# Retention, feed-forward and expert attention in one kernel: pair 0 loaded over two queues, pairs 1 and 2 scaled by GpSimd, and the last pair's mask ahead of low parts

## The chip, the cores and the metric

The kernel runs on one core of a Trainium2 chip. The metric is device time in microseconds (us), the median of several executions. A core has five engines that run their own instruction streams and meet at semaphores: TensorE (PE in the profile), VectorE (DVE), ScalarE (ACT), GpSimd (POOL) and SyncE (SP), which only issues transfers here. PEld are TensorE's weight loads. A name with q (SPq, ACTq) is an engine's own queue of issued transfers.

## The reference, cut to what matters

```python
# 1. retention: q, k, v are (2, 8, 768, 64)
gamma = 1.0 - 2.0 ** (-5.0 - np.arange(H))
for t in range(S):
    state = gamma * state + k[:, :, t] (outer) v[:, :, t]
    y[:, :, t] = 1 / sqrt(D) * q[:, :, t] @ state
# 2. feed-forward on x = y as (2, 768, 512)
xn = (x - mean) / sqrt(var + 1e-6) * g_ln
x = x + relu(xn @ w_ch1) @ w_ch2              # 512 -> 2048 -> 512
# 3. four attention experts, the best two of four by x @ w_gate
for e in range(4):
    a = softmax(causal(scale * (x @ wq[e]) @ (x @ wk[e]).T))
    out += weight_of(e) * (a @ (x @ wv[e]) @ wo[e])
```

The decay of the retention is moved into q and k: row t of q is multiplied by gamma^t / sqrt(D) and row t of k by gamma^-t (t counted from the middle), so that the rest is a causal product without decay.

## The kernel before

**Pairs.** The 16 (batch, head) combinations are worked as 8 pairs of two heads (`NIT` = 8, `HP` = 4 of each batch), a pair as 6 chunks of 128 rows in two halves `g` of three chunks. For a pair `it`:

- `load_heads(it)` on SyncE: k, q and v, 384 KB each, into one of three buffers (`RB`). From pair 3 on, k and q wait until the scaling of pair it - 3 is done, and v until its outputs are.
- `scale_rows` (L295): one half of k or q times its column of the table `decay`, a multiplication with two inputs in SBUF. VectorE does pairs 0 and 1 and q of pair 2; GpSimd does the rest in `scale_pair`, in the order k, q of half 0 and k, q of half 1. They wait for `s_tab_rest`, the rest of the table.
- `turn` (TensorE, L614): three transposes for each of four units, k and q of half 0, k and q of half 1, each into a PSUM bank; `turned` (ScalarE, L960) evacuates one unit into `k_t` or `q_t`.
- `scores_of` (L624): 6 products for a half; `apply_causal` (VectorE, L1176) masks them into `prob`.
- `key_values` (L671): k times v of chunks 0 to 4; `states` (VectorE, L1185 and L1188) adds them up, one copy and four additions, each waiting for the one before.
- `chunk_outputs` (L637) and `state_outputs` (L644): both add into the pair's output banks; `y_out` (ScalarE, L966) takes them to `x`, already transposed.

Products in fp32 are two instructions each in the profile, except the transposes. TensorE's order is written out by hand: in steady state scores(it), chunk_outputs(it - 1), key_values(it), state_outputs(it - 1), turn(it + 1).

**Front.** Pair 0 comes in pieces by half and head: `FIRST` is k0, q0, k1, q1, v0, v1, each two pieces of 96 KB. SyncE issues the first table (12 KB), the head-0 pieces of k0 and q0, both pieces of the others, then the rest of the table, which holds seven pairs although the values of both batches are equal, then pair 1. ScalarE issues the head-1 pieces of k0 and q0. TensorE meanwhile does 18 transposes (L677) that nobody reads. VectorE's order is: scale pair 0, `apply_causal(0, 0)`, `states(0)`, `apply_causal(0, 1)`, scale pair 1.

**Into the feed-forward block.** It works in float32r parts, hi and lo of each operand, and takes three of the four products: `PASSES` is (hi, hi), (hi, lo), (lo, hi), the first of each the weight and the second the activation. The inner loop of `hidden` (L727) needs the normalised x: `first_sum` (L1240, L1244) adds the four pairs of a batch into `head_sum`, `first_mean` (TensorE, L654) makes the mean, `first_centre` (L1250) subtracts it, `first_hi` (ScalarE, L978) writes the hi part and `first_lo` (VectorE, L1256) the lo part. `first_centre(b, kk)`, `first_hi` and `first_lo` exist for two batches `b` and four blocks `kk` of 128. Those of batch 0 are done during pairs 6 and 7, those of batch 1 after the last pair. `hidden(0, 0)` waits block by block for the lo part of batch 1.

**Last pairs.** TensorE's order there is scores(7), key_values(7), chunk_outputs of half 0 of pairs 6 and 7, their state_outputs, chunk_outputs of half 1 of both, `first_mean(1)`, state_outputs of half 1 of both, `hidden(0, 0)`. After it come the feed-forward block, in three stages of 16 `hidden` and 16 `project` (L736), and the attention, both in TensorE's hand-written order, up to the end.

Of the kernel before, what the change touches and what calls it, by code (L numbers as in the profile page):

```python
# [32 lines left out]
P = 128  # L33
# [3 lines left out]
FAR = 3e38  # L37


def decay_tables(heads, seq, head_dim, batch):  # L40


    gamma = 1.0 - 2.0 ** (-5.0 - np.arange(heads, dtype=np.float64))
    t = np.arange(seq, dtype=np.float64).reshape(seq // P, P) - seq // 2
    power = gamma[None, None, :] ** t[:, :, None]
    both = np.stack([power / np.sqrt(head_dim), 1.0 / power])
    both = both.reshape(2, seq // P, P, heads // 2, 2).transpose(2, 0, 3, 1, 4)
    both = both.reshape(P, 2, heads // 2, -1)
    return np.concatenate([both] * batch, axis=2).astype(np.float32)


class Chain:
# [18 lines left out]
def retention_moe_program(nc, q, k, v, g_ln, w_ch1, w_ch2, w_gate, wq, wk, wv, wo, out):  # L71
    B, H, S, D = q.shape
    DM, FF = w_ch1.shape
    E = w_gate.shape[1]
    HP = H // 2
    NIT = B * HP
# [8 lines left out]
    G = 3  # L85
# [4 lines left out]
    assert B == 2 and D == 64 and DM == H * D == 512 and NC == 6 and E * D == 2 * P and N == 512  # L90

    heads = {n: a.rearrange("b (i j) (c p) d -> (b i) p j c d", j=2, p=P) for n, a in (("q", q), ("k", k), ("v", v))}
    tables = nc.inline_tensor(decay_tables(H, S, D, B), name="decay")
    w1_rows = w_ch1.rearrange("(k p) f -> p k f", p=P)
    w2_rows = w_ch2.rearrange("(f p) n -> p f n", p=P)
    gate_rows = w_gate.rearrange("(k p) e -> p k e", p=P)
# [5 lines left out]
    with ExitStack() as ctx:  # L102
        def sb(scope, name, shape, dt=F32):
            return scope.enter_context(nc.sbuf_tensor(name, shape, dt))

        def sem(name):
            return ctx.enter_context(nc.semaphore(name))
# [6 lines left out]
        mean_of = sb(ctx, "mean_of", [P, P], F32R)  # L114
        causal = sb(ctx, "causal", [P, P])
        masked = sb(ctx, "masked", [P, NC, P], BF16)
        decay = sb(ctx, "decay_sb", [P, 2, NIT, 2 * NC])
        rvar = sb(ctx, "rvar", [P, NT])
        g_col = sb(ctx, "g_col", [P, KT])

# [80 lines left out]
        s_const = sem("s_const")  # L201
        s_tab, s_tab_rest = sem("s_tab"), sem("s_tab_rest")
        s_wraw, s_gcol = sem("s_wraw"), sem("s_gcol")
        s_first = {n: [sem(f"s_first_{n}{g}") for g in range(2)] for n in "qkv"}
        s_load = {n: [sem(f"s_load_{n}{m}") for m in range(RB)] for n in "qkv"}
        s_scaled = {n: sem(f"s_scaled_{n}") for n in "qk"}

# [33 lines left out]
        s_done = [sem(f"s_done{n}") for n in range(3)]  # L241


        PASSES = (("hi", "hi"), ("hi", "lo"), ("lo", "hi"))

        def f32(ap):
# [32 lines left out]
        def part_of(g):  # L279
            return slice(G * g, G * g + G)  # L280

        FIRST = (("k", 0), ("q", 0), ("k", 1), ("q", 1), ("v", 0), ("v", 1))

        def wait_loaded(engine, n, which, g):

            if n == 0:
                engine.wait_ge(s_first[which][g], 32)
            else:
                engine.wait_ge(s_load[which][n % RB], 16 * (n // RB + (n % RB > 0)))

        def scale_rows(engine, n, which, g):

            wait_loaded(engine, n, which, g)
            factors = decay[:, "qk".index(which), n, 2 * G * g:2 * G * (g + 1)].rearrange("p (c j) -> p c j", j=2)
            engine.tensor_tensor(scaled[which][:, n % RB, part_of(g)].rearrange("p c (j d) -> p c j d", j=2),  # L295
                                 raw[which][:, n % RB, :, part_of(g)].rearrange("p j c d -> p c j d"),
                                 factors.unsqueeze(3).broadcast_to((P, G, 2, D)),
                                 ALU.mult).then_inc(s_scaled[which], 1)
# [101 lines left out]
        def _(sp):  # L400
# [38 lines left out]
                    sp.dma_start(f32(k_twice["lo"][j * D:(j + 1) * D, e % 2, b, cols]),  # L439
                                 f32(pj["lo"][D:2 * D, n % 2, :])).then_inc(s_spread[n % 2], 16)  # L440

            sp.dma_start(decay[:, :, 0:1, :], tables[:, :, 0:1, :]).then_inc(s_tab, 16)
            for n, g in FIRST:
                for j in range(1 if (n, g) in FIRST[0:2] else 2):
                    sp.dma_start(raw[n][:, 0, j, part_of(g)], heads[n][0][:, j, part_of(g)]).then_inc(s_first[n][g], 16)
            sp.dma_start(decay[:, :, 1:NIT, :], tables[:, :, 1:NIT, :]).then_inc(s_tab_rest, 16)
            for it in range(1, NIT):
                load_heads(it)
                if it == RB:
# [26 lines left out]
        def _(pool):  # L476
# [34 lines left out]
            def scale_pair(n):  # L511

                for g in range(2):
                    for which in "kq"[0:1 if n == 2 else 2]:
                        if g == 0 and (n, which) in ((2, "k"), (3, "q")):
                            pool.wait_ge(s_scaled[which], 2 * n)
                        if n == 2 and g == 0:
                            pool.wait_ge(s_tab_rest, 16)
                        if n >= RB and g == 0:
                            pool.wait_ge(s_t, 4 * (n - RB) + 4)  # L520
                            if which == "k":
                                pool.wait_ge(s_kv, n - RB + 1)
                        scale_rows(pool, n, which, g)

            for n in range(2, NIT):
                scale_pair(n)
            split_w1(0)
            split_w1(1)
# [76 lines left out]
        def _(pe):  # L605
# [33 lines left out]

            def state_outputs(it, g):  # L640

                pe.wait_ge(s_st, (NC - 1) * (it + 1))
                for c in range(max(1, G * g), G * g + G):
                    mm = pe.matmul(y_bank(it, g)[:, (c - G * g) * P:(c - G * g + 1) * P], state[:, it % 2, c - 1, :],  # L644
                                   q_t[:, it % 2, c, :], start=False, stop=True, skip_group_check=True)
                mm.then_inc(s_y, 1)
# [28 lines left out]
            pe.wait_ge(s_const, 2)  # L675
            for _ in range(18):
                pe.transpose(ps[:, 5, 0:P], ident[:, :], ident[:, :])  # L677
            for unit in range(4):
                turn(0, unit)
                if unit == 1:  # L680
                    scores_of(0, 0)
            key_values(0)
            scores_of(0, 1)
            for g in range(2):
                chunk_outputs(0, g)
                state_outputs(0, g)
            for unit in range(4):
                turn(1, unit)
            for it in range(1, NIT - 1):

                for g in range(2):
                    scores_of(it, g)
                if it > 1:
                    for g in range(2):
                        chunk_outputs(it - 1, g)
                key_values(it)
                if it > 1:
                    for g in range(2):
                        state_outputs(it - 1, g)
                for unit in range(4):  # L700
                    turn(it + 1, unit)
                if it == HP + 1:
                    first_mean(0)
# [14 lines left out]
            def hidden(i, f):  # L718
                pe.wait_ge(s_w1, f + 1)
                if f >= 2:  # L720

                    pe.wait_ge(s_hlo, NF * i + f - 1)
                for kk in range(KT):
                    if f == 0:
                        pe.wait_ge(s_xlo, KT * (i + 1) + kk + 1)
                    for p_, (a_, b_) in enumerate(PASSES):
                        mm = pe.matmul(ps[:, f % 2, :], w1[a_][:, f, kk, :], xn_t[b_][:, kk, :],  # L727
                                       start=(kk == 0 and p_ == 0), stop=(kk == KT - 1 and p_ == 2))
                mm.then_inc(s_h, 1)
# [221 lines left out]
        def _(act):  # L951
# [31 lines left out]
            act.wait_ge(s_const, 2)  # L983

            act.activation(rvar[:, :], ident[:, 0:NT], ACT.Sqrt).then_inc(s_preload, 1)
            for unit in range(4):
                turned(0, unit)
            for it in range(1, NIT):
                if it == HP + 3:
                    for kk in range(KT):  # L990
                        first_hi(0, kk)
                if it != 2:
                    for g in range(2):
                        y_out(max(0, it - 2), g)
                for unit in range(4):
                    turned(it, unit)
            for it in (NIT - 2, NIT - 1):
                y_out(it, 0)
            for kk in range(KT):
# [169 lines left out]
        def _(dve):  # L1169
# [26 lines left out]
            dve.wait_ge(s_preload, 1)  # L1196
            dve.wait_ge(s_const, 4)
            apply_causal(0, 0)
            states(0)
            apply_causal(0, 1)  # L1200
            dve.wait_ge(s_tab_rest, 16)
            for g in range(2):
                for n in "kq":
                    scale_rows(dve, 1, n, g)

            def normalise(n):

# [142 lines left out]
            for it in range(1, NIT):  # L1350
                if it == HP + 2:
                    for kk in range(KT):
                        first_centre(0, kk)
                if it == HP + 3:
                    for kk in (2, 3):
                        first_lo(0, kk)
                b, kk = divmod(it - 2, HP)
                if it >= 2 and kk > 0:
                    first_sum(b, kk)
                apply_causal(it, 0)  # L1360
                if it < NIT - 1:
                    apply_causal(it, 1)
                if it == 1:
                    for g in range(2):
                        scale_rows(dve, 2, "q", g)
                states(it)
                if it == HP + 2:
                    for kk in (0, 1):
                        first_lo(0, kk)
            apply_causal(NIT - 1, 1)  # L1370
            first_sum(1, HP - 2)
            first_sum(1, HP - 1)
            first_centre(1, 0)
# [191 lines left out]
```

## Time and profile before

| | |
|---|---|
| median of 3 runs | 468.07 us (467.91 to 468.2) |
| the profiled execution | 467.95 us |
| its span, first to last instruction | 466.2 us |
| TensorE busy in the span | 453.8 us, 97% |
| VectorE, ScalarE, GpSimd busy | 272.1, 149.6, 151.9 us |
| granted TensorE clock, mean | 1.00 |

The profile is of one execution. Times in its views count from the start of the span. "Busy" counts an instruction from start to end, and TensorE's overlap, so a busy TensorE is not one without waits; the chain of waits and the timeline tell more. In the timeline [idle before <-releaser] is how long the engine had stood idle and what ended that; rows that follow one another without a pause are merged, with their number behind the x.

### The profile page before, as it was taken

How to read it: one execution, taken by the hardware profiler on the slowest of the kernel's cores; microseconds unless marked ns; L12 is line 12 of the kernel's file. 1: busy time of each engine (PE TensorE's matmuls, PEld its weight loads, DVE VectorE, ACT ScalarE, POOL GpSimd, SP SyncE). 2: the span in 40 equal slices, each digit the busy share in tenths (PEclk: the TensorE clock that was granted, in tenths of full speed). 3: DMA queues.
4: the chain of work that ended last, by engine and by line, in shares of the span. 5: the costliest groups of instructions: out<-in, count | busy, mean ns of one | idle time of the engine just before them, and what ended most of it. 6: DMA issues, size and time to landing. Idle time of an engine off the chain costs nothing.

```text
span 466.2 us, 7435 instructions
## 1 busy us (share of the span) xinstructions
PE 453.8 (97%) x2762; PEld 393.0 (84%) x2762; DVE 272.1 (58%) x601; ACT 149.6 (32%) x343; POOL 151.9 (33%) x188
## 2 busy tenths in 40 slices
PE   7999999999999999999999999999999999999896
PEld 6899888888888888888888888888999899998775
DVE  4765941385416388732265784144538889888833
ACT  2344431111212111111121111141435777777823
POOL 1264449999600000000002000001402567666710
PEclk9999999999999999999999999999999999999999
DMA  7997415444000000000040000000155444442024
GB/s 170 248 218 180 125 46 136 135 135 136 22 1 1 0 0 0 0 0 0 0 112 3 0 1 0 0 2 0 24 136 123 113 123 105 99 105 63 1 112 159
DMA packets 65792, 33.04 MB, mean 71 GB/s; under 512 B 47584, under 2 KB 61920, under 8 KB 65760
## 3 DMA queue, kind: packets, MB, share of 16 engines
q1 hardware_dynamic: 64960, 32.43, 26.9%
q8 instruction: 19, 0.31, 0.3%
q10 hardware_dynamic: 800, 0.20, 0.2%
q14 instruction: 13, 0.11, 0.1%
HBM read 20.03 MB, written 3.15 MB: 50 GB/s over the span
## 4 chain that ended last, share of the span: by engine, by line
PE 86%; DVE 7%; ACT 2%; issue 2%; POOL 1%; DMA 0%; POOLq 0%; ACTq 0%; DVEq 0%
PE ps L727 28%; PE ps L736 28%; PE ps L811 5%; PE ps L862 4%; PE ps L783 3%; PE ps L830 3%; PE ps L845 2%; PE ps L889 2%; PE ps L637 2%; PE ps L624 2%; PE ps L614 2%; DVE a L1445 2%; PE ps L644 2%; DVE a_low_lo L1453 1%; PE ps L677 1%
## 5 line engine op out<-in xcount | busy, mean ns | idle before, releaser
L1296 DVE SCALAR_TENSOR_TENSOR h_t_lo<-ps,h_t_hi 128x512 fp32r<-128x512 f32 x48 | 33.2, 692 | 124.4 <-ACT h_t_hi L1012 124.4
L1012 ACT ACTIVATE h_t_hi<-ps 128x512 fp32r<-128x512 f32 x48 | 28.7, 598 | 216.2 <-PE ps L727 216.2
L727 PE MATMUL ps<-xn_t_hi,w_hi 128*128 128x512 f32 x192 | 74.9, 390 | 0.3 <-DVE xn_t_lo L1256 0.3
L727 PE MATMUL ps<-xn_t_lo,w_hi 128*128 128x512 f32 x192 | 74.8, 390 | 0.0
L727 PE MATMUL ps<-xn_t_hi,w_lo 128*128 128x512 f32 x192 | 74.8, 390 | 0.0
L736 PE MATMUL ps<-w_hi,h_t_lo 128*128 128x512 f32 x192 | 74.8, 390 | 0.0
L736 PE MATMUL ps<-w_lo,h_t_hi 128*128 128x512 f32 x192 | 74.8, 389 | 0.0
L736 PE MATMUL ps<-w_hi,h_t_hi 128*128 128x512 f32 x192 | 74.8, 389 | 0.0
L575 POOL TENSOR_SCALAR a<-a,inv_den,weight 128x768 f32<-128x768 f32 (+5 forms) x48 | 33.9, 716 | 50.5 <-DVE inv_den L1465 50.2
L727 PEld LDWEIGHTS ps<-xn_t_hi,w_hi 128*128 128x128 f32 x192 | 36.1, 188 | 8.4 <-issue 0.5
L736 PEld LDWEIGHTS ps<-w_hi,h_t_hi 128*128 128x128 f32 x192 | 36.0, 188 | 7.5
L736 PEld LDWEIGHTS ps<-w_lo,h_t_hi 128*128 128x128 f32 x192 | 36.0, 188 | 7.5
L727 PEld LDWEIGHTS ps<-xn_t_hi,w_lo 128*128 128x128 f32 x192 | 36.0, 188 | 7.5
L736 PEld LDWEIGHTS ps<-w_hi,h_t_lo 128*128 128x128 f32 x192 | 36.1, 188 | 7.4
L727 PEld LDWEIGHTS ps<-xn_t_lo,w_hi 128*128 128x128 f32 x192 | 36.1, 188 | 7.3
L538 POOL TENSOR_SCALAR w_vg_hi<-raw_vg 128x1040 fp32r<-128x1040 f32 x1 | 1.1, 1060 | 120.4 <-DMA raw_wo<-in_moe_wo 120.4
L1067 ACT ACTIVATE a<-a,neg_max 128x768 f32<-128x768 f32 (+5 forms) x48 | 32.3, 674 | 13.8 <-DVE neg_max L1445 13.8
L1283 DVE STREAM_TRANSPOSE rows<-x 32x512 f32<-32x512 f32 x48 | 33.7, 702 | 1.4
L1445 DVE CUSTOM_DVE_ANT_0 a<-ps,masked 128x768 f32<-128x768 f32 (+5 forms) x48 | 27.8, 617 | 0.3 <-PE ps L830 0.3
L845 PE MATMUL ps<-ident,a 128*128 128x128 f32 x168 | 23.6, 277 | 3.5 <-DVE a_low_lo L1453 2.4
L546 POOL TENSOR_SCALAR raw_qk<-raw_qk 128x256 f32<-128x256 f32 x4 | 1.6, 406 | 76.9 <-PE ps L736 76.0
L845 PEld LDWEIGHTS ps<-ident,a 128*128 128x128 f32 x168 | 18.6, 141 | 6.5 <-POOL a L575 5.0
(146 smaller groups left out, 889.1 us busy)
## 6 DMA issues: line engine op xcount, KB each, us to landing
raw_w<-in_moe_w_ch SPq DMA_DIRECT2D x32, 256.0 KB, 2.9
k_twice_hi<-pj_hi SPq DMA_DIRECT2D x32, 96.0 KB, 2.2
k_twice_lo<-pj_lo SPq DMA_DIRECT2D x32, 96.0 KB, 2.2
out_y<-out_sb SPq DMA_DIRECT2D x12, 256.0 KB, 2.0
raw_k<-in_k SPq DMA_DIRECT2D x7, 384.0 KB, 4.5
raw_q<-in_q SPq DMA_DIRECT2D x7, 384.0 KB, 4.9
raw_v<-in_v SPq DMA_DIRECT2D x7, 384.0 KB, 3.4
q_both<-pj_hi SPq DMA_DIRECT2D x16, 96.0 KB, 2.1
```

Source lines behind the costliest of these rows:

```text
L575: pool.tensor_scalar(a[:, g % AB, c0:c1], a[:, g % AB, c0:c1], inv_den[:, u:u + 1], weight[:, u, e:e + 1], ALU.mult, ALU.mult).then_inc(s_ ...
L727: mm = pe.matmul(ps[:, f % 2, :], w1[a_][:, f, kk, :], xn_t[b_][:, kk, :], start=(kk == 0 and p_ == 0), stop=(kk == KT - 1 and p_ == 2))
L736: mm = pe.matmul(ps[:, 2 + tau, :], h_t[a_][:, f % 2, tau * P:(tau + 1) * P], w2[b_][:, f, :], start=(f == 0 and p_ == 0), stop=(f == NF - ...
L783: mm = pe.matmul(v_bank(t), x2[a_][:, b, kk, c * P:(c + 1) * P], w_vg[b_][:, kk, :], start=(kk == 0 and p_ == 0), stop=(kk == KT - 1 and p ...
L811: mm = pe.matmul(pj_bank(n), w_qk[a_][n // 4 % 2][:, kk, :], x2[b_][:, b, kk, half_cols(n)], start=(kk == 0 and p_ == 0), stop=(kk == KT - ...
L845: mm = pe.transpose(flat(4, 6, s0 + P)[:, s0:s0 + P], a[:, g % AB, s0:s0 + P], ident[:, :])
L862: mm = pe.matmul(z_bank(top)[:, skip:HALF], ev[:, b * NC + sc, e].rearrange("p h d -> p (h d)"), (a_top if top else a_low)[part][:, sc, sk ...
L1012: act.activation(h_t["hi"][:, f % 2, :], ps[:, f % 2, :], ACT.Relu).then_inc(s_hhi, 1)
L1067: act.activation(a[:, g % AB, c0:c1], a[:, g % AB, c0:c1], ACT.Exp, bias=neg_max[:, 2 * (g % AB) + w:2 * (g % AB) + w + 1], scale=-1.0, ac ...
L1283: dve.transpose(rows[quad(a_), :, :, :, quad(d_)].rearrange("p b k u d -> p (b k) u d"), x[quad(d_), :, U * n:U * n + U, quad(a_)]).then_i ...
L1296: dve.scalar_tensor_tensor(h_t["lo"][:, f % 2, :], ps[:, f % 2, :], 0.0, f32(h_t["hi"][:, f % 2, :]), ALU.max, ALU.subtract).then_inc(s_hl ...
L1445: dve.tensor_tensor_reduce(a[:, g % AB, c0:c1], sc_bank(g, c1)[:, c0:c1], masked[:, NC - 1 - i:NC, :].rearrange("p c t -> p (c t)"), -1.0, ...
```

## The change

Four things are done:

- **Loads.** v of pair 0 is issued by ScalarE, behind its first activation, in two pieces of 192 KB, one for each head, under one semaphore `s_first_v`. The first table goes behind the first piece of k. The table holds four pairs, used by both batches (`n % HP`), so that the rest is 36 KB where it was 84.
- **Scaling.** GpSimd scales all of pairs 1 and 2 too.
- **Order of pairs 0 and 1.** `scores_of(0, 0)` goes behind the third unit of `turn(0)`; `apply_causal(0, 1)` ahead of `states(0)`; `turn(1)` ahead of `state_outputs(0)`; ScalarE's `y_out(0)` behind `turned(1)`. `state_outputs` waits only for the states that its half reads.
- **Last pair.** `apply_causal(7, 0)` goes ahead of two of the low parts of batch 0 and of the sum of pairs 4 and 5; one low part comes behind it, and the other and the sums after the last mask. The first product of a feed-forward stage (`f == 0`) takes the passes hi-hi, lo-hi, hi-lo and waits for the hi part of a block, and for its lo part only ahead of the third pass.

```diff
-def decay_tables(heads, seq, head_dim, batch):
+def decay_tables(heads, seq, head_dim):
...
-    both = both.reshape(P, 2, heads // 2, -1)
-    return np.concatenate([both] * batch, axis=2).astype(np.float32)
+    return both.reshape(P, 2, heads // 2, -1).astype(np.float32)
...
+        LATE_LOW = (("hi", "hi"), ("lo", "hi"), ("hi", "lo"))
...
-        FIRST = (("k", 0), ("q", 0), ("k", 1), ("q", 1), ("v", 0), ("v", 1))
+        FIRST = (("k", 0), ("q", 0), ("k", 1), ("q", 1))
...
-                engine.wait_ge(s_first[which][g], 32)
+                engine.wait_ge(s_first_v if which == "v" else s_first[which][g], 32)
...
@@ SyncE @@
-            sp.dma_start(decay[:, :, 0:1, :], tables[:, :, 0:1, :]).then_inc(s_tab, 16)
             for n, g in FIRST:
                 for j in range(1 if (n, g) in FIRST[0:2] else 2):
                     sp.dma_start(raw[n][:, 0, j, part_of(g)], heads[n][0][:, j, part_of(g)]).then_inc(s_first[n][g], 16)
-            sp.dma_start(decay[:, :, 1:NIT, :], tables[:, :, 1:NIT, :]).then_inc(s_tab_rest, 16)
+                if (n, g) == FIRST[0]:
+                    sp.dma_start(decay[:, :, 0:1, :], tables[:, :, 0:1, :]).then_inc(s_tab, 16)
+            sp.dma_start(decay[:, :, 1:HP, :], tables[:, :, 1:HP, :]).then_inc(s_tab_rest, 16)
...
@@ GpSimd @@
-                    for which in "kq"[0:1 if n == 2 else 2]:
-                        if g == 0 and (n, which) in ((2, "k"), (3, "q")):
-                            pool.wait_ge(s_scaled[which], 2 * n)
-                        if n == 2 and g == 0:
-                            pool.wait_ge(s_tab_rest, 16)
+                    for which in "kq":
+                        if n == 1 and g == 0:
+                            pool.wait_ge(s_scaled[which], 2)
...
-            for n in range(2, NIT):
+            pool.wait_ge(s_tab_rest, 16)
+            for n in range(1, NIT):
                 scale_pair(n)
...
@@ TensorE @@
-                pe.wait_ge(s_st, (NC - 1) * (it + 1))
+                pe.wait_ge(s_st, (NC - 1) * it + G * g + G - 1)
...
-            for unit in range(4):
+            for unit in range(3):
                 turn(0, unit)
-                if unit == 1:
-                    scores_of(0, 0)
+            scores_of(0, 0)
+            turn(0, 3)
             key_values(0)
             scores_of(0, 1)
             for g in range(2):
                 chunk_outputs(0, g)
-                state_outputs(0, g)
             for unit in range(4):
                 turn(1, unit)
+            for g in range(2):
+                state_outputs(0, g)
...
-                        pe.wait_ge(s_xlo, KT * (i + 1) + kk + 1)
-                    for p_, (a_, b_) in enumerate(PASSES):
+                        pe.wait_ge(s_xhi, KT * (i + 1) + kk + 1)
+                    for p_, (a_, b_) in enumerate(LATE_LOW if f == 0 else PASSES):
+                        if f == 0 and b_ == "lo":
+                            pe.wait_ge(s_xlo, KT * (i + 1) + kk + 1)
...
@@ ScalarE @@
             act.activation(rvar[:, :], ident[:, 0:NT], ACT.Sqrt).then_inc(s_preload, 1)
+            for j in range(2):
+                act.dma_start(raw["v"][:, 0, j], heads["v"][0][:, j]).then_inc(s_first_v, 16)
...
-                if it != 2:
+                if it > 2:
                     for g in range(2):
-                        y_out(max(0, it - 2), g)
+                        y_out(it - 2, g)
                 for unit in range(4):
                     turned(it, unit)
+                if it == 1:
+                    for g in range(2):
+                        y_out(0, g)
...
@@ VectorE @@
             apply_causal(0, 0)
+            apply_causal(0, 1)
             states(0)
-            apply_causal(0, 1)
-            dve.wait_ge(s_tab_rest, 16)
-            for g in range(2):
-                for n in "kq":
-                    scale_rows(dve, 1, n, g)
...
-                if it == HP + 3:
-                    for kk in (2, 3):
-                        first_lo(0, kk)
                 b, kk = divmod(it - 2, HP)
-                if it >= 2 and kk > 0:
+                if 2 <= it < NIT - 1 and kk > 0:
                     first_sum(b, kk)
                 apply_causal(it, 0)
                 if it < NIT - 1:
                     apply_causal(it, 1)
-                if it == 1:
-                    for g in range(2):
-                        scale_rows(dve, 2, "q", g)
+                else:
+                    first_lo(0, 2)
                 states(it)
...
             apply_causal(NIT - 1, 1)
+            first_lo(0, 3)
+            first_sum(1, HP - 3)
             first_sum(1, HP - 2)
```

## Rows read from the trace of the kernel before

**Rows 1.** Busy time by stretch; columns: stretch, engines, clock, DMA share, GB/s.
```profile
0.00:5.70 5.70, 4.12 (x20) 4.12 (x21) 1.71 (x3) 1.49 (x2) 2.25 (x11) 1.00 0.56 122
5.70:14.00 8.30, 7.11 (x89) 5.78 (x89) 5.99 (x13) 2.23 (x5) 0.00 (x0) 1.00 1.04 235
9.10:12.50 3.40, 3.19 (x48) 2.58 (x48) 2.41 (x8) 0.44 (x2) 0.00 (x0) 1.00 1.20 274
14.00:21.80 7.80, 7.29 (x97) 6.31 (x95) 5.15 (x11) 3.77 (x9) 2.43 (x3) 1.00 1.04 236
```

**Rows 2.** The chain that ended last, first 33 us: start, us, what.
```profile
1.58 4.10 PE ps L677 x18
...
9.11 0.82 PE ps L671 x20
...
11.46 0.96 DVE prob L1176
...
18.45 0.54 DVE scaled_q L295
...
19.03 1.20 PE ps L614 x9
...
28.27 1.46 PE ps L637 x24
29.73 0.58 PE ps L671 x20
30.31 1.31 PE ps L644 x10
31.62 1.31 PE ps L614 x12
...
32.96 1.70 PE ps L624 x24
```

**Rows 3.** Timeline of the front: start, us, engine, line, operation, [idle before].
```profile
3.08 0.20 ACT L985 ACTIVATE rvar<-ident 128x4 f32<-128x4 f32 x1
...
4.93 2.09 SPq L445 DMA_DIRECT2D raw_v<-in_v  x4
...
7.01 0.56 DVE L295 TENSOR_TENSOR scaled_q<-raw_q,decay_sb 128x384 f32<-128x384 f32 x1 [0.68 <-DMA raw_q<-in_q]
...
7.64 0.60 SPq L409 DMA_DIRECT2D raw_k<-in_k  x1
...
12.26 1.28 SPq L409 DMA_DIRECT2D raw_q<-in_q  x1
...
16.94 1.62 POOL L295 TENSOR_TENSOR scaled_k<-raw_k,decay_sb 128x384 f32<-128x384 f32 x2 [13.65 <-DMA raw_k<-in_k]
```

**Rows 4.** The DMA view: issues at 7.64 and 12.26; the last column is us to landing.
```profile
raw_k<-in_k SPq DMA_DIRECT2D x1, 384.0 KB, 3.8
...
raw_q<-in_q SPq DMA_DIRECT2D x1, 384.0 KB, 5.9
```

**Rows 5.** Timeline of the last pairs and of the feed-forward block's first product.
```profile
51.31 3.23 DVE L1256 SCALAR_TENSOR_TENSOR xn_t_lo<-centred,g_col,xn_t_hi 128x256 fp32r<-128x256 f32 x4
...
52.40 1.71 PE L624 MATMUL ps<-q_t,k_t 64*128 64x128 f32 x24
...
54.79 0.95 DVE L1176 TENSOR_TENSOR prob<-ps,causal 128x768 f32<-128x768 f32 x1
...
57.16 0.95 DVE L1176 TENSOR_TENSOR prob<-ps,causal 128x768 f32<-128x768 f32 x1
...
58.02 0.97 DVE L1244 TENSOR_TENSOR head_sum<-head_sum,x 128x256 f32<-128x256 f32 x2
...
59.39 0.70 PE L654 MATMUL ps<-head_sum,mean_of 128*128 128x256 f32 x2
...
61.13 0.48 DVE L1256 SCALAR_TENSOR_TENSOR xn_t_lo<-centred,g_col,xn_t_hi 128x256 fp32r<-128x256 f32 x1 [0.25 <-ACT xn_t_hi L978]
...
61.76 0.47 PE L727 MATMUL ps<-xn_t_hi,w_hi 128*128 128x512 f32 x1 [0.33 <-DVE xn_t_lo L1256]
```

More of the change, by code:

```diff
@@ L92, in retention_moe_program @@
     heads = {n: a.rearrange("b (i j) (c p) d -> (b i) p j c d", j=2, p=P) for n, a in (("q", q), ("k", k), ("v", v))}
-    tables = nc.inline_tensor(decay_tables(H, S, D, B), name="decay")
+    tables = nc.inline_tensor(decay_tables(H, S, D), name="decay")
     w1_rows = w_ch1.rearrange("(k p) f -> p k f", p=P)
@@ L116, in retention_moe_program @@
         masked = sb(ctx, "masked", [P, NC, P], BF16)
-        decay = sb(ctx, "decay_sb", [P, 2, NIT, 2 * NC])
+        decay = sb(ctx, "decay_sb", [P, 2, HP, 2 * NC])
         rvar = sb(ctx, "rvar", [P, NT])
@@ L203, in retention_moe_program @@
         s_wraw, s_gcol = sem("s_wraw"), sem("s_gcol")
-        s_first = {n: [sem(f"s_first_{n}{g}") for g in range(2)] for n in "qkv"}
+        s_first = {n: [sem(f"s_first_{n}{g}") for g in range(2)] for n in "qk"}
+        s_first_v = sem("s_first_v")
         s_load = {n: [sem(f"s_load_{n}{m}") for m in range(RB)] for n in "qkv"}
@@ L293, in scale_rows @@
             wait_loaded(engine, n, which, g)
-            factors = decay[:, "qk".index(which), n, 2 * G * g:2 * G * (g + 1)].rearrange("p (c j) -> p c j", j=2)
+            factors = decay[:, "qk".index(which), n % HP, 2 * G * g:2 * G * (g + 1)].rearrange("p (c j) -> p c j", j=2)
             engine.tensor_tensor(scaled[which][:, n % RB, part_of(g)].rearrange("p c (j d) -> p c j d", j=2),
```

## The prediction

> **What bounds the kernel now.** I read the page first: the profiled execution took 467.95 us, of which the span is 466.2, so 1.75 us lie around it; the median of the three timed runs is 468.07. I make the sum in span time and take it off 468.07. TensorE is busy almost throughout, and at 1.00 of its clock in each stretch that I looked at. So a change pays only where TensorE's chain has waits. The stretches of the front [rows 1] show where: 7.11 of 8.30 us busy, then 7.29 of 7.80, and in the first 5.7 us the DMA engines are only 0.56 busy while the SyncE queue hands out small pieces. From 9.1 us they are full, at 274 GB/s.
>
> The chain [rows 2] orders it. Warm-up transposes hold TensorE from 1.58 to 5.68. Key-value products of pair 0 start at 9.11; the mask of the second half (11.46) and the scaling of pair 2's q on VectorE (18.45) stand in the chain, and pair 2 is turned by 19.03 + 1.20 = 20.23. From there TensorE alone is left: outputs 1.46, key-values 0.58, state outputs 1.31, turning 1.31, scores 1.70, together 6.36 us a pair. Until 52.4 there is no wait worth pursuing. The last stretch [rows 5] has two: TensorE waits behind mask (7,0), which starts only at 54.79 behind four low-part products, and the first feed-forward product starts at 61.76, released by a low part. Both ends of the first stage, then, and all that follows is TensorE's own chain and moves with them one for one.
>
> **The change, part by part: the front.** Pair 0's v moves from four SyncE pieces to two ScalarE ones. The four took 2.09 us of the SyncE queue [rows 3], so pair 1's k is issued at about 5.5 instead of 7.64, q and v behind it. Putting the first decay table behind k's first piece shifts nothing: q's first piece and both k pieces behind it keep their places, and the first transposes are held by the warm-up, which ends at 5.68. The table of the rest shrinks from seven pairs to three.
>
> ScalarE issues v after its activation at 3.08, so at 3.3 to 4.5, before its first evacuation is due after 5.7. The v halves now share the DMA engines with q's second half, which VectorE scaled at 7.01. About 340 KB of q and k were then still to come; at half of 274 GB/s that is 2.5 us instead of some 2.0, so I put that scaling at 7.4 (bounds 7.0 and 7.8). Turning it ends near 8.5, v is there by about 7.7, and the key-values run at 8.5 instead of 9.11.
>
> Then TensorE, with durations of [rows 2]: key-values to 9.2; scores of the second half (half of 1.70) to 10.1; mask 10.15 to 11.1, now ahead of the states; second output half (half of 1.46) 11.2 to 11.95; turning pair 1 to 13.3; state outputs of pair 0, now behind it, to 14.6; scores 16.3; key-values 16.9; turning pair 2 to 18.25. The chain before had 20.23 there. **Bound by TensorE, the front gains 1.9 us.**
>
> The other side is the feed. GpSimd now scales pairs 1 and 2. Two of its scalings take 1.62, so each about 0.83 and the next 0.79 later [rows 3]; VectorE's take 0.56. They take k, q, k, q, so three stand behind the landing of q: 0.05 + 0.79 + 0.79 + 0.83 = 2.46 us, then 0.13 to wake TensorE and a quarter of the turning, 0.33: turned about 2.9 us after q lands. Before: landing at 12.26 + 5.9 = 18.2 [rows 3, 4] and 20.23, so 2.05. The move costs 0.9 us wherever the data come last, and VectorE has nothing else that it was holding up. When does pair 2's q land? Pair 1's k landed at 7.64 + 3.8 = 11.4 [rows 4]. All bytes up to it, now 1.62 MB, are the same but 48 KB. By 5.7 us 122 GB/s x 5.7 = 0.70 MB had moved [rows 1]; two queues filling the idle part of the engines from about 4.4 on add some 0.12. The 0.80 MB left need 2.9 us at 274 and 3.4 at 235 GB/s, which with half a microsecond to the semaphore is 9.1 to 9.6; I take 9.4. Four more transfers of 0.39 MB follow: 5.7 us at 274 GB/s, but 6.8 as they took before (11.4 to 18.2). So q lands at 15.1 to 16.2, and pair 2 is turned at 18.0 to 19.1. With 18.25 from TensorE's side the front gains 1.9 or 1.1; nothing in the profile says which transfer will be slow, so I take the middle: **1.5 us**. Pair 1 by the same rule has q at 10.8 and its last unit at 13.7, some 0.4 behind TensorE's own 13.3, which is inside that span.
>
> GpSimd's scaling is 1.5 times VectorE's in the trace, 0.83 against 0.56 [rows 3]. The Trainium skill (GPSIMD Engine Reference, Engine selection) says that two-input elementwise work is about twice as slow there and belongs on VectorE; by it each would be 1.1 us. The row decides, and the rest is a rival below.
>
> **The tail.** Scores of pair 7 start at 52.40, so their first half is done near 53.4, and mask (7,0) starts there instead of at 54.79. Ahead of it are now only two low parts, done by 51.31 + half of 3.23 = 52.9. From that mask's start to the other mask's end took 57.16 + 0.95 - 54.79 = 3.32; one low part of 0.48 goes between: ends at 57.2. (The four at 51.31 took 0.81 each and the later one 0.48; GpSimd was splitting weights beside the four, and is done by then.) Then come the last low part and three sums, 0.48 + 3 x 0.485 = 1.93: head sum complete at 59.1, mean at about 59.2, against 59.39. TensorE is ready earlier: 52.4 + 1.70 + 0.58 + 1.46 + 1.05 (8 of 10 state matmuls of [rows 2]) + 1.46 = 58.65, and waits 0.5. The sums that moved behind the masks are now what is late.
>
> From mean to first product took 61.76 - 59.39 = 2.37, its last link the low part's 0.48. With the high passes first, that link goes, and then both TensorE (mean 0.35 plus 12 state matmuls at 1.31 / 10 each, 1.57: 1.92) and the high part (1.75) are ready at 1.9 to 2.0. First product at 61.2: **0.5 us** (bounds: 0.2, only the mean's; and 0.8, were the sums to overlap). Low parts stay ahead: each costs centre plus low, about 0.75 against 0.70 us of TensorE, with some 0.4 in hand.
>
> Sum: 1.5 + 0.5 = 2.0, 468.07 - 2.0 = 466.1 us.
>
> **Rivals.**
> *Data-bound front.* v takes from q and k what it saves, so pair 2's q comes at most 1.2 us earlier, 17.0. Then it is turned at 19.9, a gain of 0.3 in front; with 0.5 behind, 467.3 us. For it: from 9.1 us the engines are full. Against: 0.56 before 5.7, room that the new queue can use. With a gain of 1.6 in q's landing it would be 466.9. The Trainium skill (DMA: Bandwidth & Descriptors, Issuing engines are not separate DMA queues) says that a second issuing engine saves issue time only, since all share 16 engines; by that rule this rival gains weight as the engines fill.
> *GpSimd slower than its row.* Beside a VectorE that is busy with masks, a scaling might take twice VectorE's 0.56, so 1.12. Three then stand 0.9 us longer behind q: 466.1 + 0.8 = 466.9. Against: GpSimd's pair of scalings at 16.94 ran beside two masks, in 0.83 each. By the rule of the Trainium skill cited above (GPSIMD Engine Reference, Engine selection) this would be the case.
> *A later wait takes it.* Pair 3's q lands about three transfers after pair 2's, 4.1 to 4.3, so its last unit is scaled at 16.2 + 4.3 + 2.46 = 23.0 and TensorE wants it at 18.75 + 1.70 + 1.46 + 0.58 + 1.31 + 1.0 = 24.8; slack 1.8, so this needs another slow transfer. If it eats the whole front gain: 467.6, no change.
> *Slower: ScalarE stuck in its issues.* The v issues stand ahead of the first evacuation on ScalarE. SyncE's issue takes 0.60 for pair 1's k and 1.28 for pair 2's q [rows 3] when the queue is full. If the two v issues end past 6.1, all of pair 0 moves by the excess, and the excess costs the end as soon as it is over the 2.0 gained: past 8.1, 2.4 us an issue. At 2.8 each they end at 8.9, and the time is 468.9. Against: at 3.3 us little is in flight.
>
> **How the numbers follow.** A measurement here tells about 0.2%, 0.94 us, from no change; below 467.1 is faster. Forecast (front 1.1 to 1.9, tail 0.2 to 0.7: 465.5 to 466.8) 0.6; data-bound 0.18, half of it under 467.1; GpSimd slower than its row 0.04; later wait 0.1, same; slower side 0.08, of it 0.06 by over 0.2%. Faster 0.60 + 0.09 + 0.04 + 0.02 for the late wait eating only part = 0.75; same 0.19; slower 0.06. The range for 8 in 10 takes the forecast and most of the data-bound case, with a little under the best sum: 465.3 to 467.4.
>
> **What would show it.** After: k of pair 1 issued at about 5.5 and landed by 9.8; key-values of pair 0 at 8.5; GpSimd's last scaling of pair 2 ended before 18.7; pair 2 turned between 18.2 and 19.1 against 20.23; then the same 6.4 us a pair; mask (7,0) 1.4 us earlier in its pair; TensorE waiting some 0.5 for the mean; first product released by a high part, 2.0 behind the mean. It is wrong if ScalarE's first evacuation comes after 6.2, if v's halves hold the second q half past 7.8, if TensorE waits at pair 1 or 2 for GpSimd by over 1 us, or if a wait appears at pair 3 or 4.

## The result

The changed kernel takes 469.31 us (12 runs, 468.0 to 470.49) against 468.13 us (12 runs): the ratio is 1.0026, its 95% interval 1.0017 to 1.0035, so it is slower by 1.2 us, where 2.0 us less was forecast. Its profiled execution took 468.87 us with a span of 466.9.

The stretches of the front, of the changed kernel, columns as in [rows 1] (the DMA share adds up the times of the packets, so it passes 1 where packets overlap in an engine):

```profile
5.70:14.00 8.30, 6.71 (x82) 5.03 (x82) 4.66 (x9) 1.96 (x4) 2.26 (x3) 1.00 1.35 216
9.10:12.50 3.40, 3.40 (x59) 2.81 (x57) 1.70 (x3) 0.80 (x2) 0.83 (x1) 1.00 1.35 218
14.00:21.80 7.80, 6.95 (x78) 5.55 (x76) 3.48 (x9) 4.15 (x9) 4.21 (x6) 1.00 1.25 220
```

TensorE has less to do in the last stretch, 6.95 of 7.80 us where it had 7.29. And the DMA engines are busier than before and move less: from 9.1 to 12.5 us a share of 1.35 gives 218 GB/s, where 1.20 gave 274.

The chain of waits of the changed kernel:

```profile
11.48 7.34 DMA raw_q<-in_q
...
18.89 0.83 POOL scaled_q L296
19.72 0.79 POOL scaled_k L296
20.50 0.80 POOL scaled_q L296
...
21.35 0.55 PE ps L615 x3
21.90 1.54 PE ps L625 x24
```

Pair 2 is turned at 21.35 + 0.55 = 21.90, against 19.03 + 1.20 = 20.23 in [rows 2]: 1.67 us later. The chain behind it runs through three scalings of GpSimd, 0.83 and two of 0.8, back to the transfer of pair 2's q, issued at 11.48. Its landing and that of pair 1's k, in the DMA view:

```profile
raw_k<-in_k SPq DMA_DIRECT2D x1, 384.0 KB, 5.3
...
raw_q<-in_q SPq DMA_DIRECT2D x1, 384.0 KB, 7.3
```

So pair 1's k lands at 5.36 + 5.3 = 10.7 (before: 11.4 [rows 3, 4]) and pair 2's q at 11.48 + 7.3 = 18.8 (before: 18.2). The SyncE queue is 2.3 us ahead at pair 1's k, and 0.7 of it is left when that lands; four transfers later it is 0.6 behind. From one to the other are 8.1 us for what took 6.8.

The start, in the timeline of the changed kernel:

```profile
1.90 1.28 ACT L989 ACT_TABLE_LOAD   x1 [1.90 <-issue]
1.96 1.04 ACTq L991 DMA_DIRECT2D raw_v<-in_v  x2
...
3.19 0.21 ACT L989 ACTIVATE rvar<-ident 128x4 f32<-128x4 f32 x1
...
5.36 0.60 SPq L410 DMA_DIRECT2D raw_k<-in_k  x1
...
6.05 0.56 DVE L296 TENSOR_TENSOR scaled_q<-raw_q,decay_sb 128x384 f32<-128x384 f32 x1 [0.98 <-DMA raw_q<-in_q]
...
8.81 0.94 PE L625 MATMUL ps<-q_t,k_t 64*128 64x128 f32 x12
...
10.15 0.80 PE L672 MATMUL ps<-raw_v,scaled_k 128*64 128x64 f32 x20
```

ScalarE issues v at 1.96, while the table load of its activation is still running and the activation itself is yet to come (3.19 to 3.40). So v's 384 KB go among the first pieces of q and k, not behind them: q of half 0 is scaled only from 6.05, the first scores start at 8.81, and the key-values at 10.15, against 9.11 in [rows 2].

The end of the first stage, in the timeline of the changed kernel:

```profile
53.98 1.71 PE L625 MATMUL ps<-q_t,k_t 64*128 64x128 f32 x24
...
54.97 0.96 DVE L1185 TENSOR_TENSOR prob<-ps,causal 128x768 f32<-128x768 f32 x1 [0.86 <-PE ps L625]
...
57.97 0.95 DVE L1185 TENSOR_TENSOR prob<-ps,causal 128x768 f32<-128x768 f32 x1
...
59.75 0.95 DVE L1249 TENSOR_TENSOR head_sum<-head_sum,x 128x256 f32<-128x256 f32 x2
...
60.85 0.67 PE L655 MATMUL ps<-head_sum,mean_of 128*128 128x256 f32 x2 [0.57 <-DVE head_sum L1249]
...
62.56 0.48 DVE L1261 SCALAR_TENSOR_TENSOR xn_t_lo<-centred,g_col,xn_t_hi 128x256 fp32r<-128x256 f32 x1 [0.25 <-ACT xn_t_hi L982]
...
62.67 0.47 PE L731 MATMUL ps<-xn_t_hi,w_hi 128*128 128x512 f32 x1
```

From the scores of pair 7 to the first product are 62.67 - 53.98 = 8.69 us, against 61.76 - 52.40 = 9.36 in [rows 5]: 0.67 us gained. Mask (7,0) starts 0.99 behind the scores instead of 2.39; TensorE waits 0.57 for the sums ahead of the mean; the first product starts while the low part of its block is still being made. The two numbers add up: + 1.67 - 0.67 = + 1.0, and the profiled executions differ by 0.92.

The 9.36 is of one execution. In the second profile of the kernel before (`e1`, below) the same stretch took 61.34 - 52.46 = 8.88 us; the changed tail took 8.68 to 8.70 in every profile that shows it:

```profile
52.46 1.70 PE L624 MATMUL ps<-q_t,k_t 64*128 64x128 f32 x24
...
61.34 0.47 PE L727 MATMUL ps<-xn_t_hi,w_hi 128*128 128x512 f32 x1 [0.33 <-DVE xn_t_lo L1256]
```

So what the tail is worth rests on the timed runs of `e8`, not on this pair of rows.

### The profile page after: what moved, and what is told of

It reads as the page before. It is cut to its first block, busy times and chain, and to the rows that moved or that the text cites. A ratio compares the mean times of both kernels' runs of the same rounds, so it can differ in the third digit from the quotient of the medians.

```text
span 466.9 us, 7433 instructions
## 1 busy us (share of the span) xinstructions
PE 453.8 (97%) x2762; PEld 392.5 (84%) x2762; DVE 266.6 (57%) x595; ACT 150.1 (32%) x343; POOL 156.5 (34%) x194
## 4 chain that ended last, share of the span: by engine, by line
PE 84%; DVE 6%; SPq 2%; DMA 2%; ACT 2%; issue 2%; POOL 1%; POOLq 0%; DVEq 0%; ACTq 0%
PE ps L731 28%; PE ps L740 28%; PE ps L815 5%; PE ps L866 4%; PE ps L787 3%; PE ps L834 3%; PE ps L849 2%; PE ps L893 2%; PE ps L625 2%; DVE a L1448 2%; PE ps L645 2%; DMA raw_q<-in_q 2%; PE ps L638 2%; PE ps L615 2%; SPq L410 1%
```

## The experiments

**Is it the kernel or the chip?** Four kernels ran on one chip: before and changed, each again, and two that put v elsewhere. `e1` and `e2` are the two kernels unchanged.

> The kernel before, profiled a second time beside the changed one. The question is the transfer rate: from 10 to 14 us the first profile had 285 GB/s here and 217 in the changed kernel, with fewer bytes. Theory 1 (the change lowers the rate): 280 or more from 10 to 14 us, pair 2 turned at 20.2 us. Theory 2 (the rate belongs to the chip or to the execution): it can be 217 here, with pair 2 turned later than 21. Time 468.1 by the first, up to 1.5 more by the second.

> The changed kernel a second time, on the same chip. Theory 1: again near 217 GB/s from 8 to 18 us, q of pair 2 scaled first at 18.9, time 469.3. Theory 2: the rate equals that of the kernel before on this chip.

`e3` puts v back on SyncE:

```diff
-            for j in range(2):
-                act.dma_start(raw["v"][:, 0, j], heads["v"][0][:, j]).then_inc(s_first_v, 16)
...
-        FIRST = (("k", 0), ("q", 0), ("k", 1), ("q", 1))
+        FIRST = (("k", 0), ("q", 0), ("k", 1), ("q", 1), ("v", 0), ("v", 1))
```

> The changed kernel with v of pair 0 back on SyncE in four pieces behind q, as before; the rest of the change stays. Theory 1a (v on the second queue, ahead of q and k, is the cause): q of pair 0 scaled at 4.9 again, key-values at 9.1, rate 280, q of pair 2 landing at 18 or earlier; scaled by GpSimd, pair 2 is turned near 20.9; with the tail's 0.7 gained the time is 468.0 or a little less. Theory 2 (rate of the chip): as slow as the changed kernel, 469.

`e4` holds ScalarE's issue until its activation is done:

```diff
+            act.wait_ge(s_preload, 1)
             for j in range(2):
                 act.dma_start(raw["v"][:, 0, j], heads["v"][0][:, j]).then_inc(s_first_v, 16)
```

> The changed kernel, ScalarE waiting for its activation to finish before it issues v, so at 3.4 us and not at 1.96. Theory 1b (it is v ahead of q and k that costs, not the second queue): q of pair 0 scaled at 4.9, scores of the first half at 7.2 where the changed kernel has 8.81; time 467 to 468. If the rate afterwards is low only because two queues are used, pair 2 is still turned past 21.

| kernel | median us | ratio to before, 95% interval |
|---|---|---|
| before | 468.13 | |
| e1 before again | 467.85 | 0.9999 (0.9989 to 1.0009) |
| e2 changed again | 468.92 | 1.0020 (1.0010 to 1.0030) |
| e3 v on SyncE | 469.37 | 1.0027 (1.0017 to 1.0037) |
| e4 v waits | 468.57 | 1.0009 (0.9999 to 1.0018) |

The slow transfers belong to the kernel: `e1` has them fast and `e2` slow on the same chip. They do not come from v's place: `e3` keeps them, with v on SyncE as before, and its median is the highest of the four. Theory 1a fell. In `e4` q of half 0 is scaled at 4.72 and the first scores start at 7.27, and its median is 0.35 us under that of `e2`, with intervals that overlap; but pair 2 is turned at 21.87, hardly earlier than in the changed kernel. What `e2`, `e3` and `e4` share and `e1` lacks are the order of work, the scaling on GpSimd, and a smaller table. The stretch from 14 to 18 us, first of `e1`:

```profile
14.00:18.00 4.00, 3.97 (x60) 3.59 (x59) 1.66 (x3) 2.02 (x5) 1.62 (x2) 1.00 1.17 265
```

and of the changed kernel:

```profile
14.00:18.00 4.00, 3.95 (x46) 3.59 (x44) 0.68 (x3) 2.68 (x6) 1.81 (x3) 1.00 1.32 222
```

Dividing the last column by the one before it gives what the engines move while busy: 265 / 1.17 = 226 GB/s against 222 / 1.32 = 168. It isn't only that transfers come at other times; on the average of this stretch each packet takes 1.35 times as long. The table offers a reason. It lies in SBUF ahead of everything that the transfers write, and it is 384 bytes a partition shorter. The builds give the addresses: raw_q, raw_k and raw_v start at 130048, 139264 and 148480 before, multiples of 512, and at 129664, 138880 and 148096 in the changed kernel, 128 past one. They are written in rows of 256 bytes (64 numbers), so that every row now crosses a multiple of 256.

**The address alone, both ways.** `e5` is the changed kernel with the old addresses, `e7` the kernel before with 128 bytes more behind the table:

```diff
@@ e5, on the changed kernel @@
         decay = sb(ctx, "decay_sb", [P, 2, HP, 2 * NC])
+        sb(ctx, "rest_of_table", [P, 2, HP, 2 * NC])
@@ e7, on the kernel before @@
         decay = sb(ctx, "decay_sb", [P, 2, NIT, 2 * NC])
+        sb(ctx, "shift", [P, P // 4])
```

> The changed kernel with 384 bytes a partition left free behind the halved table, so that every later tile has the address that it had before: raw_q, raw_k and raw_v at a multiple of 512 bytes, where the changed kernel has them 128 bytes past one. Nothing else differs. Theory A (address: rows of 256 bytes written at 128 past a boundary are slower): full-rate stretches at 270 GB/s or more instead of 217, q of pair 2 landing at 15 to 16.5 instead of 18.8, time 466 to 467.4. Theory B (fewer bytes, the queues or the order of issues set the rate): 217 GB/s again and 469.

> The kernel before, with 128 bytes a partition inserted behind the table, so that raw_q, raw_k and raw_v start 128 bytes past a multiple of 256. Nothing else differs. Theory A: the full-rate stretches fall from 275 to about 217 GB/s, q of pair 2 lands 1.5 to 2 us later (at 20), and the time rises by 1.0 to 2.5 us, to 469 to 470.5. Theory B: no difference, 468.1.

`e6` is `e5` with the wait of `e4`:

> As the run before, and ScalarE waits for its activation ahead of the issues of v, so that v goes at 3.4 us, behind the first pieces of q and k. Theory A: q of pair 0 scaled at 4.9 instead of 6.0, rate 270 or more, pair 2 turned at 18.3 to 19.2; the best of all versions, 466.1, and 0.3 to 1.0 under the run before if pair 0 then bounds. If pair 2's q bounds, the two are equal.

`e11` and `e12` are `e7` with 256 and 64 bytes:

```diff
@@ e11 @@
-        sb(ctx, "shift", [P, P // 4])
+        sb(ctx, "shift", [P, 64])
@@ e12 @@
-        sb(ctx, "shift", [P, P // 4])
+        sb(ctx, "shift", [P, 16])
```

> The kernel before, tiles moved by 256 bytes: raw tiles at a multiple of 256 but not of 512. If a row of 256 bytes must only not cross a 256-byte boundary: no difference, 468.1, and 255 GB/s or more from 10 to 14 us. If the boundary that counts is 512: half the rows or all would be slow, 468.8 or more.

> The kernel before, tiles moved by 64 bytes: each row of 256 bytes crosses a 256-byte boundary, as in the 128-byte shift, which gave 469.6 and 221 GB/s from 14 to 18 us. If each row is cut in two pieces at the boundary: the same, 469 to 470.5. If only a 128-byte offset hurts: 468.1.

The stretch from 14 to 18 us in `e5`, in `e7` and in `e12`:

```profile
14.00:18.00 4.00, 4.00 (x61) 3.69 (x59) 1.28 (x2) 2.25 (x6) 3.18 (x4) 1.00 1.17 265
```

```profile
14.00:18.00 4.00, 3.96 (x60) 3.58 (x58) 2.07 (x4) 2.02 (x5) 0.88 (x2) 1.00 1.33 221
```

```profile
14.00:18.00 4.00, 4.00 (x59) 3.43 (x57) 2.48 (x5) 2.02 (x5) 0.00 (x0) 1.00 1.26 209
```

| kernel | raw tiles past a multiple of 256 | GB/s, DMA share, 14 to 18 us | GB/s by share | median us | ratio, 95% interval |
|---|---|---|---|---|---|
| e1 before again | 0 | 265, 1.17 | 226 | 467.85 | 0.9999 (0.9989 to 1.0009) |
| e11 before, 256 on | 0 | 252, 1.12 | 225 | 468.33 | 0.9995 (0.9981 to 1.0009) |
| e12 before, 64 on | 64 | 209, 1.26 | 166 | 470.01 | 1.0039 (1.0024 to 1.0054) |
| e7 before, 128 on | 128 | 221, 1.33 | 166 | 469.60 | 1.0025 (1.0016 to 1.0034) |
| changed | 128 | 222, 1.32 | 168 | 469.31 | 1.0026 (1.0017 to 1.0035) |
| e5 changed, old addresses | 0 | 265, 1.17 | 226 | 467.03 | 0.9968 (0.9955 to 0.9980) |
| e6 the same, v waits | 0 | 239, 1.05 | 228 | 466.81 | 0.9964 (0.9951 to 0.9978) |

Theory A holds in both directions. One empty tile makes the changed kernel 1.2 us faster than before instead of 1.2 us slower; one empty tile makes the kernel before 1.3 us slower. A step of 256 bytes does nothing; 64 bytes hurt no less than 128. The engines' own work does not change with the addresses: a scaling takes 0.83 us on GpSimd and 0.56 on VectorE in the changed kernel and in `e5`.

The rows are not slow from the start. One microsecond each of `e7`:

```profile
10.00:11.00 1.00, 1.00 (x18) 0.88 (x18) 0.86 (x3) 0.00 (x0) 0.00 (x0) 1.00 1.27 285
...
12.00:13.00 1.00, 0.76 (x10) 0.59 (x11) 0.99 (x2) 0.49 (x1) 0.00 (x0) 1.00 1.35 218
...
20.00:21.00 1.00, 0.30 (x2) 0.31 (x3) 0.92 (x2) 0.00 (x0) 0.00 (x0) 0.96 1.05 242
```

285 / 1.27 = 224 is the rate of the old addresses, 218 / 1.35 = 161 is slow, and behind a pause (a share of 0.50 from 19 to 20 us) it is 242 / 1.05 = 230 again. Before 10 us `e7` shows nothing of its shift: from 6 to 10 it has 186 / 0.83 = 224, and pair 1's k lands 3.9 us behind its issue, as in `e1`. So the address costs only where the engines have been kept full for a while. The changed kernel fills them earlier, with v on the second queue: 274 / 1.23 = 223 from 4 to 5 us, but 218 / 1.35 = 161 already from 6 to 7. Why the cost sets in late, no run tells.

The chain of `e5`:

```profile
9.12 0.48 PE ps L616 x3
...
13.22 1.46 PE ps L616 x12
...
18.07 1.46 PE ps L616 x12
19.53 1.68 PE ps L626 x24
```

Pair 2 is turned at 19.53, against 20.23 in [rows 2] and 21.90 in the changed kernel, and from 7.1 us on no transfer stands in this chain, only TensorE's work, one scaling of VectorE and a mask. In `e6` v is out of the way of q's first half, as its timeline shows, but not of the second:

```profile
3.43 0.98 ACTq L993 DMA_DIRECT2D raw_v<-in_v  x2
...
4.67 0.55 DVE L297 TENSOR_TENSOR scaled_q<-raw_q,decay_sb 128x384 f32<-128x384 f32 x1
...
8.06 0.56 DVE L297 TENSOR_TENSOR scaled_q<-raw_q,decay_sb 128x384 f32<-128x384 f32 x1 [1.33 <-DMA raw_q<-in_q]
...
9.15 0.80 PE L673 MATMUL ps<-raw_v,scaled_k 128*64 128x64 f32 x20
...
19.12 0.55 PE L616 MATMUL ps<-ident,scaled_q 128*128 128x128 f32 x3 [0.19 <-POOL scaled_q L297]
```

q of half 0 is scaled at 4.67, that of half 1 only at 8.06, and key-values come at 9.15. TensorE then waits 0.19 for GpSimd's last scaling of pair 2. `e6` and `e5` are not told apart by their intervals; `e6` has the lowest median of all, and both beat both kernels.

**What the other parts are worth, with the old addresses.** `e9` is `e5` with v on SyncE (the edit of `e3`); `e10` is `e5` with VectorE scaling pair 1 and pair 2's q:

```diff
             apply_causal(0, 1)
             states(0)
+            dve.wait_ge(s_tab_rest, 16)
+            for g in range(2):
+                for n in "kq":
+                    scale_rows(dve, 1, n, g)
...
+                if it == 1:
+                    for g in range(2):
+                        scale_rows(dve, 2, "q", g)
                 states(it)
```

> The changed kernel with the old addresses and with v of pair 0 on SyncE as before. What v's own move is worth. By the prediction's step (v off SyncE brings pair 1 and 2 in 2.1 us earlier) this version loses most of the front: q of pair 2 near 18.2, three GpSimd scalings behind it, pair 2 turned near 21.1, time 468.3. By the rival (v's sharing costs pair 0 what it saves later) it is equal to the padded change, 467.0.

> The changed kernel with the old addresses, and VectorE scaling pair 1 and q of pair 2 as before. What the move to GpSimd costs. By the prediction it costs 0.9 us only where the data come last; in the padded change TensorE waited for a GpSimd scaling 0.2 us, so at most 0.3 us faster, 466.7 to 467.3. If VectorE's scalings now hold masks or states, slower by their four times 0.56, up to 468.

`e9` takes 468.14 us, 0.9996 (0.9984 to 1.0008): 1.1 us more than `e5`. Its chain:

```profile
11.96 5.84 DMA raw_q<-in_q
...
17.87 0.83 POOL scaled_q L296
...
20.33 0.55 PE ps L615 x3
```

q of pair 2 lands at 17.8, against 10.66 + 4.9 = 15.6 in `e5`, and the turning ends 3.08 behind it. So v's move is what brings the data 2.2 us forward, and it carries the front's whole gain; the rival that v takes from q and k what it saves is wrong for pair 2 once the rows lie right. (How early the data come differs by execution: pair 2's q landed at 18.2, 17.4, 18.3 and 18.8 in the profiles of the kernel before, `e1`, `e8` and `e11`, and at 15.6, 16.6 and 17.1 in `e5`, `e6` and `e10`. The two groups don't meet.)

`e10` takes 469.40 us, 1.0034 (1.0014 to 1.0054): 2.4 us more than `e5` by the medians. I had expected at most 0.3 less, or up to 468 if the scalings held masks or states. Its timeline:

```profile
11.66 0.96 DVE L1186 TENSOR_TENSOR prob<-ps,causal 128x768 f32<-128x768 f32 x1 [1.02 <-PE ps L626]
...
14.03 0.55 DVE L297 TENSOR_TENSOR scaled_k<-raw_k,decay_sb 128x384 f32<-128x384 f32 x1
...
14.64 0.55 PE L616 MATMUL ps<-ident,scaled_k 128*128 128x128 f32 x3 [1.00 <-DVE scaled_k L297]
...
18.62 1.82 DVE L1186 TENSOR_TENSOR prob<-ps,causal 128x768 f32<-128x768 f32 x2 [2.64 <-PE ps L626]
...
20.36 1.21 DVE L297 TENSOR_TENSOR scaled_q<-raw_q,decay_sb 128x384 f32<-128x384 f32 x2
...
21.16 0.55 PE L616 MATMUL ps<-ident,scaled_q 128*128 128x128 f32 x3 [0.70 <-DVE scaled_q L297]
```

VectorE comes to pair 1 only at 14.03, behind the mask at 11.66 and the states, and to pair 2's q at 20.36, behind two masks. TensorE waits 1.00 and 0.70 us for it, although pair 2's q had landed at 10.59 + 6.5 = 17.1. The kernel before comes to pair 1 at 12.33:

```profile
12.33 0.55 DVE L295 TENSOR_TENSOR scaled_k<-raw_k,decay_sb 128x384 f32<-128x384 f32 x1
```

Its masks and states stood ahead of the scaling too, but the states ran between the two masks. The change puts them behind the second one, so that VectorE comes to the scaling 1.7 us later, and it turns pair 1 ahead of the state outputs, so that TensorE wants it 0.5 us earlier (14.64 - 1.00 = 13.64, against 14.13). In this order the move to GpSimd is not a cost that hides; it is needed. Not all of the 2.4 us is its worth: in the profile of `e10` the key-values of pair 0 already come 0.4 us later than in `e5` (9.94 against 9.53), and 4 of its 12 executions had a lower mean clock (0.991 to 0.996); the other eight have a median of 469.1.

`e8` is the kernel before with the last part alone:

```diff
-                if it == HP + 3:
-                    for kk in (2, 3):
-                        first_lo(0, kk)
                 b, kk = divmod(it - 2, HP)
-                if it >= 2 and kk > 0:
+                if 2 <= it < NIT - 1 and kk > 0:
...
+                if it == NIT - 1:
+                    first_lo(0, 2)
                 states(it)
...
             apply_causal(NIT - 1, 1)
+            first_lo(0, 3)
+            first_sum(1, HP - 3)
```

and the order of passes of the change.

> The kernel before with the last part of the change alone: mask (7,0) ahead of two low parts, sums behind the last mask, first product in the order hi-hi, lo-hi, hi-lo. In the changed kernel it took 8.69 us from the scores of pair 7 to the first product instead of 9.36. So 0.6 to 0.7 us faster, 467.4; if what is gained there is given back in the low parts of the first product, 467.8 or more.

It takes 467.62 us, 0.9984 (0.9975 to 0.9994): 0.65 us under the median of the kernel before on the same chip (468.27). From the scores of pair 7 to the first product are 8.69 us, as in the changed kernel:

```profile
52.33 1.70 PE L625 MATMUL ps<-q_t,k_t 64*128 64x128 f32 x24
...
61.02 0.47 PE L730 MATMUL ps<-xn_t_hi,w_hi 128*128 128x512 f32 x1
```

## Why the prediction was wrong

**The step that failed is the landing of pair 2's q**, put at 15.1 to 16.2 from 274 GB/s, or 231 as before. It landed at 18.8, because with the engines full the rows went at 218 GB/s: from 14 to 18 us each took 1.35 times as long. The prediction took the smaller table for a matter of bytes alone ("the same but 48 KB") and never asked what lies behind it in SBUF. With the addresses as they were, pair 1's k landed at 5.36 + 3.9 = 9.3 (`e5`), forecast 9.4 (the half microsecond to the semaphore in that sum stands in no row), and pair 2's q at 15.6 (`e5`), inside the forecast, and at 16.6 (`e6`) and 17.1 (`e10`), outside it. No rival held the cause. The data-bound one had its mechanism right (the transfers decide, three GpSimd scalings stand behind them) and priced it at 467.3 with v as the culprit; `e3` and `e9` cleared v. Two of the prediction's own signs of being wrong came: q's second half of pair 0 was scaled only at 8.65 (it named 7.8), and ScalarE's first evacuation began at 6.36 (it named 6.2).

**ScalarE's issue time.** "ScalarE issues v after its activation at 3.08" was read off the order in the code. The issue doesn't wait for the activation: 1.96, not 3.3 to 4.5. That made pair 0 late. The wait is worth 0.35 us in `e4` (against `e2`) and 0.22 in `e6` (against `e5`), less than their intervals, since the transfers behind are what ends last in both.

**The scaling on GpSimd.** "About 2.9 us after q lands" was right: 18.8 to 21.90 is 3.1, and `e9` has 3.08. "The move costs 0.9 us wherever the data come last, and VectorE has nothing else that it was holding up" was half wrong: in the new order VectorE has, and without the move the kernel loses some 2 us (`e10`). Nor did the data come last in the kernel before: in `e1` pair 2's q landed at 12.34 + 5.1 = 17.4 instead of 18.2, and pair 2 was turned no earlier, at 20.29, because VectorE was at its masks until 18.57. The 2.05 us that the prediction put between landing and turning hold some of that wait.

**The tail** was forecast at 0.5, within 0.2 to 0.8: 0.67 between the first two profiles, 0.65 alone in timed runs (`e8`, interval 0.3 to 1.2). The mean came 60.85 - 53.98 = 6.87 us behind the scores, forecast 59.2 - 52.4 = 6.8; from mean to first product 1.82, forecast 2.0.

**What is left.** With addresses right, 466.8 to 467.0 is 0.7 to 0.9 above the forecast: the front gains 20.23 - 19.53 = 0.7 in `e5`, forecast 1.5. TensorE's own chain was priced well: from the key-values to the turned pair 2 it took 19.53 - 9.60 = 9.9 us in `e5`, forecast 18.25 - 8.5 = 9.75. What was late is where it starts, pair 0. In `e6` q's second half is scaled at 8.06, forecast 7.4, and key-values come at 9.15, forecast 8.5; behind that only 0.19 us is a wait for GpSimd. That v still shares with q's second half, for longer than half the rate would give, is argued and not shown; v behind that half wasn't tried.

**The two levels of the clock** were no part of the forecast and took a part in the result. The stretches of the changed kernel and of `e5` shown here are at 1.00, the 2.4 GHz level. But 8 of the 12 timed executions of the changed kernel have a mean granted clock of 0.993 to 0.996, and 7 of 10 in `e2`; of `e1`, `e4`, `e5` and `e6` none has. The profile of `e2` shows where:

```profile
8.82 0.56 PE L615 MATMUL ps<-ident,scaled_k 128*128 128x128 f32 x3 [1.51 <-DVE scaled_k L296]
9.32 1.65 PE L625 MATMUL ps<-q_t,k_t 64*128 64x128 f32 x12
...
10.00:11.00 1.00, 1.00 (x11) 0.78 (x10) 0.00 (x0) 0.00 (x0) 0.00 (x0) 0.50 1.22 215
```

TensorE had waited 0.63 and 1.51 us in pair 0, and then its clock was at 0.50, the 1.2 GHz level, from about 9.2 to 12.6 us; the scores took 1.65 us, where the changed kernel's profile has 0.94. Pair 2's q landed at 11.88 + 6.4 = 18.3 in `e2`, earlier than in that profile, and still pair 2 was turned only at 22.13, by TensorE's own late chain. In the profile of `e7`, the slowest of its twelve executions (470.77), TensorE waits 2.02 us for pair 2's q and the clock is at 0.50 from 20.9 to 24.3. So late data can cost twice, by the wait and by the clock behind it. How the 1.2 us divide between the two wasn't separated; the four executions of the changed kernel at 0.999 or more took 468.00, 468.84, 468.87 and 470.24.

## What to carry to other kernels

A change of a tile's size moves every tile behind it. When it is made for bytes or for order, look at the addresses that the transfers write before pricing anything: rows of 256 bytes want a multiple of 256 where the engines are kept full. In the profile the sign is GB/s divided by the DMA share: from 14 to 18 us it held within 225 to 228 for every kernel with the old addresses or 256 bytes on, and fell to 166 to 173 for the shifted ones, whatever else was changed (`e3` 168, `e2` 173). Take a stretch with a share above 1.2 that has lasted for a while: from 6 to 10 us the shifted `e7` has 224.

A part that looks like a cost by itself can be what a reordering stands on. Undo it inside the change, not only in the kernel before.

## What the runs showed of the hardware

Packets of transfers from HBM in rows of 256 bytes took 1.35 times as long (14 to 18 us, 225 to 228 against 166 to 173 GB/s by share) when the rows in SBUF started 64 or 128 bytes past a multiple of 256, and not when they started at a multiple of 256 that is none of 512 (`e11`, 225). The shifted rows were slow only with the engines full for some time: in `e7` 224 from 6 to 11 us, 161 from 12 to 13, and 230 again behind a pause. The Trainium skill (DMA: Bandwidth & Descriptors, How a descriptor splits into AXI transactions) says that a descriptor that doesn't start at a multiple of 256 starts its first transaction at the boundary below; it says so of reading. The runs agree in kind, on the writing side. By its count of beats, and this is an estimate, a row of 256 would take 10 for 8 when 64 past and 12 for 8 when 128 past; the runs show 1.36 for both. A cost for each further piece would fit that better than a cost for each beat, but neither says why the first microsecond of full engines is spared; no run settles it.

A transfer issued by ScalarE behind an activation in the program went out at 1.96 us, while the table load ran from 1.90 to 3.18 and the activation from 3.19 to 3.40. A wait on the activation's semaphore put it behind (3.43 in `e6`).

TensorE's granted clock was at 0.50 for 3.4 us behind waits of 0.63 and 1.51 us (`e2`) and behind one of 2.02 us (`e7`), and at 1.00 on both sides.
